# Expert layer in units of 256 rows, with the first layer's weights as the loaded operand

## What is computed

```python
# 1 linear attention with decay, batch 4, heads 8, 768 steps, head size 48
for t in range(S):
    cur = einsum('bhd,bhe->bhde', u*kt, vt)
    y[:, :, t] = einsum('bhd,bhde->bhe', rt, state + cur)
    state = w*state + einsum('bhd,bhe->bhde', kt, vt)
# 2 feed-forward on x [3072, 384]
h = x @ w_in                      # [384, 2048]
x = (h - tanh(h)) @ w_out         # [2048, 384]
# 3 one expert of 8 for each of the 3072 rows, by the largest cosine logit
h = maximum(x[mask] @ w1[e], 0)   # w1 [8, 384, 1024]
out[mask] = gate_w[mask] * (h @ w2[e])   # w2 [8, 1024, 384]
```

## Time and profile before

| | |
|---|---|
| median of three runs | 859.66 us |
| the profiled execution | 856.81 us |
| its span, first to last instruction | 855.0 us |
| granted TensorE clock, mean | 0.993 of 2.4 GHz |
| TensorE busy | 835.6 us (98%) |
| moved by DMA | 179.88 MB |

### The profile page before, as it was taken

One profiled execution on the slowest core, in us unless ns is written; L12 is line 12 of the kernel. 1 busy time (PEld: TensorE's weight loads), 2 busy tenths in 40 slices (PEclk: granted clock), 3 DMA queues, 4 the chain that ended last, 5 costly groups with the idle time before them and its releaser, 6 DMA issues. The chain is left out here.

```text
span 855.0 us, 18997 instructions
## 1 busy us (share of the span) xinstructions
PE 835.6 (98%) x5580; PEld 737.9 (86%) x5581; DVE 557.0 (65%) x886; ACT 481.0 (56%) x1074; POOL 283.3 (33%) x322
## 2 busy tenths in 40 slices
PE   8999989999999999999999999999999999999995
PEld 7777768889998998998998998899988999899984
DVE  8989959999999999999999997411121112111120
ACT  5666777677768777767777765133233323332331
POOL 6244434323443334434433331222222222222211
PEclk9999999999999999999999999899999999999998
DMA  8989943228779768877876986397886386411100
GB/s 245 275 256 298 281 118 95 70 89 281 240 226 298 257 218 272 277 227 257 276 238 224 305 293 226 121 335 281 306 323 249 132 308 217 172 43 46 37 2 1
DMA packets 99386, 179.88 MB, mean 210 GB/s; under 512 B 10267, under 2 KB 25773, under 8 KB 99344
## 3 DMA queue, kind: packets, MB, share of 16 engines
q1 hardware_dynamic: 92016, 163.74, 58.4%
q0 software_dynamic: 3968, 10.82, 3.8%
q10 hardware_dynamic: 3360, 4.79, 1.9%
HBM read 114.83 MB, written 65.86 MB: 211 GB/s over the span
## 5 line engine op out<-in xcount | busy, mean ns | idle before, releaser
L1205 POOL TENSOR_TENSOR ew_l<-ew_raw,ew_h 128x512 fp32r<-128x512 f32 x96 | 126.9, 1329 | 210.0 <-DVE poly L1423 205.7
L1120 PE MATMUL y_ps<-wout_h,g_h 128*128 128x392 f32 x384 | 131.3, 342 | 1.0 <-DVE g_l L1414 0.4
L1121 PE MATMUL y_ps<-wout_l,g_h 128*128 128x392 f32 x384 | 130.4, 340 | 0.0
L1122 PE MATMUL y_ps<-wout_h,g_l 128*128 128x392 f32 x384 | 130.4, 340 | 0.0
L1577 DVE TENSOR_TENSOR ex_hT_l<-e_bank,ex_hT_h 128x512 fp32r<-128x512 f32 x62 | 40.0, 686 | 125.3 <-ACT ex_hT_h L1733 125.3
L1120 PE MATMUL h_ps<-xT_h,win 128*128 (+1 forms) x288 | 113.6, 395 | 1.2 <-DVE diff L1404 0.9
L1304 ACT ACTIVATE g_h<-poly 128x512 fp32r<-128x512 f32 x96 | 61.0, 635 | 94.4 <-DVE poly L1423 93.7
L1122 PE MATMUL h_ps<-xT_h,win 128*128 (+1 forms) x288 | 113.3, 393 | 0.0
L1121 PE MATMUL h_ps<-xT_l,win 128*128 (+1 forms) x288 | 112.8, 392 | 0.0
L1733 ACT ACTIVATE ex_hT_h<-e_bank 128x512 fp32r<-128x512 f32 x62 | 33.8, 597 | 120.2 <-PE e_bank L1647 116.2
L1612 POOL DMA_INDIRECT out_dram<-ex_o_sb,put_i x31 | 31.1, 1002 | 204.1 <-ACT ex_o_sb L1717 204.1
(11 more groups left out here) (188 smaller groups left out, 1826.2 us busy)
## 6 DMA issues: line engine op xcount, KB each, us to landing
ew_raw<-in_w SPq DMA_DIRECT2D x96, 256.0 KB, 3.6
w_h<-ew_h SPq DMA_DIRECT2D x96, 256.0 KB, 3.6
w_l<-ew_l SPq DMA_DIRECT2D x96, 256.0 KB, 2.9
w_ex<-w_h SPq DMA_DIRECT2D x14, 1536.0 KB
w_ex<-w_l SPq DMA_DIRECT2D x14, 1536.0 KB
kv_sb<-in_kv SPq DMA_DIRECT2D x24, 384.0 KB, 5.8
krT_sb<-in_krT SPq DMA_DIRECT2D x44, 192.0 KB, 5.8
x_dram<-xt_sb ACTq DMA_DIRECT2D x48, 96.0 KB, 5.0
```

Source lines behind the costliest of these rows:

```text
L1120: pe.matmul(out, lh, rh, start=start, stop=False)
L1121: pe.matmul(out, lh, rl, start=False, stop=False)
L1122: return pe.matmul(out, ll, rh, start=False, stop=stop)
L1205: pool.tensor_tensor(ew_l[:, slot, :], raw, ew_h[:, slot, :].bitcast(F32), ALU.subtract).then_inc(ew_l_made, 1)
```

## The change

The feed-forward stage no longer splits the experts' first-layer weights. Only the second layer's pieces are split and stored (48 instead of 96: 8 in each middle group, 16 in the last), and `load_first` is gone.

The route builds two kinds of work: 12 **pairs** of 256 rows each and 7 **single tiles** of 128 rows. That needs more small VectorE operations between the count and the tile numbers. `expert_at` is now read by ScalarE inside the route: it loads the raw first-layer weights of pairs 0 and 1 and splits pair 0's, together with GpSimd and VectorE.

In the expert stage TensorE goes through 12 steps, one pair each (`step`). In the first layer of a pair the weights are the loaded operand and the 256 rows stream (L1841 to L1843 of the changed kernel, 72 matmuls of 256 columns). The hidden values come out with rows on columns, so that they need no transposes; ScalarE applies relu and makes the high part in one operation (`hidden_high`), VectorE the low part. The second layer is as before, twice 24 matmuls of 384 columns. Steps 1, 3, 5, 7, 9, 10 and 11 carry a single tile too, which is computed as the tiles before. Each pair's raw first-layer weights (1.5 MB) and each single tile's raw weights of both layers (3 MB) are loaded by DMAs that ScalarE issues, and are split by ScalarE and VectorE in pieces of 128x1024 while TensorE works. SP loads the split second-layer weights of all 8 experts (3 MB each) into two slots, expert 0's from the moment the gates are turned.

```diff
-FETCH = 3
+PAIR = 2 * P
+NPAIR = NT // 2
+NSOLO = E - 1
 SLOTS = 3
+SOLO_SLOT = 2
...
+def load_unit(eng, w_raw, w1, w1_loaded, e, par):
+
+    dst = w_raw[par][:, :]
+    eng.dma_start(dst.rearrange("p (a f) -> p a f", a=NP),
+                  w1[bass.ds(e * NP, NP)].rearrange("a p f -> p a f")).then_inc(w1_loaded[par], 16)
 
 
 def attention(nc, krT, kv, w, u_cols, w_in, w_outT, emb, tau, x_dram, load_group, x_sb, x_stored,
...
-    EXTRA = 4
+    PER = 8
...
             pool.wait_ge(x2_stored, 16 * NT)
             pool.wait_ge(rows_found, 1)
-            pool.indirect_dma_start(rows_sb[:, 0:DM], None, x2_dram,
-                                    bass.IndirectOffsetOnAxis(ap=get_row[:, 0:1], axis=0)).then_inc(gathered[0], 16)
+            for t in range(2):
+                pool.indirect_dma_start(rows_sb[:, t * DM:(t + 1) * DM], None, x2_dram,
+                                        bass.IndirectOffsetOnAxis(ap=get_row[:, t:t + 1],
+                                                                  axis=0)).then_inc(gathered[t], 16)
+            unit_low(pool, 1, w1_first)
...
+            act.wait_ge(h_done, KF * CH)
+            act.wait_ge(units_known, 1)
+            for u in range(2):
+                e = act.value_load(expert_at[0:1, u:u + 1], min_val=0, max_val=E - 1)
+                load_unit(act, w_raw, w1, w1_loaded, e, u)
+            act.wait_ge(w1_loaded[0], 16)
+            for n in range(SPLITS):
+                cols = slice(n * STEP, (n + 1) * STEP)
+                act.activation(unit_h[:, cols], unit_raw[:, cols], ACT.Copy).then_inc(w1_high, 1)
             act.wait_ge(shifted, 1)
             act.activation(ex[:, :, :], below[:, :, :], ACT.Exp).then_inc(ex_made, 1)
...
-            step(dve.scalar_tensor_tensor(out=base[:, :], in0=tend[:, :], scalar=ROUND, in1=ntile[:, 1, :],
-                                          op0=ALU.add, op1=ALU.subtract))
+            later(dve.tensor_scalar(ntile[:, 0, :], count_ps, 1.0 / P, (P - 1) / (2 * P), ALU.mult, ALU.add))
...
+                                    solo_at[:, :].unsqueeze(1).to_broadcast([P, E, E]), ALU.is_ge))
+            later(dve.tensor_reduce(unit_of[:, :], past[0:1, 0:NPAIR, :], AX.X, ALU.add))
+            step(dve.tensor_reduce(skipped[:, :], past_solo[:, :, :], AX.X, ALU.add))
+            dve.tensor_scalar(expert_at[:, 0:NPAIR], unit_of[:, :], float(E - 1), None, ALU.min).then_inc(units_known, 1)
+            later(dve.tensor_tensor(group_at[:, :].rearrange("p (j t) -> p j t", t=2),
+                                    tile_ids[:, :].rearrange("p (j t) -> p j t", t=2), wide(skipped[:, :], 2), ALU.add))
+            step(dve.tensor_tensor(upto[:, :, :], upto[:, :, :],
+                                   pair_rows[:, :].unsqueeze(1).to_broadcast([P, E, E]), ALU.mult))
+            step(dve.tensor_reduce(solo_group[:, :], upto[:, :, :], AX.X, ALU.add))
+            step(dve.tensor_tensor(solo_group[:, :], solo_group[:, :], solo_ids[:, :], ALU.add))
+            step(dve.copy_predicated(group_at[:, ST - E:ST], is_solo, solo_group[:, :]))
...
-            return KF if last else KF + IN_LATE if is_first(g) else KF + EXTRA
+            return KF if last else KF + IN_LATE if is_first(g) else PER
...
-                def load_first(quarter):
-                    sp.wait_ge(h_done, KF * (CH - 1) + FREED * (quarter + 1))
-                    for i in range(MADE):
-                        sp.wait_ge(ew_h_stored[i], 16 * (NP // MADE + 1))
-                        sp.wait_ge(ew_l_stored[i], 16 * (NP // MADE + 1))
-                    part, at = quarter // 2, quarter % 2
-                    for half, src in enumerate((w12_h, w12_l)):
-                        dst = w[:, 0, half, :].bitcast(F32).rearrange("p (s a q f) -> p s a q f", s=2, a=KD, f=PIECE)
-                        pieces_from = src[0:NP].rearrange("(s a q) p f -> s p a q f", s=2, a=KD)
-                        sp.dma_start(dst[:, part, :, at, :], pieces_from[part, :, :, at, :]).then_inc(first_loaded, 16)
 
                 for i in range(MADE):
...
+        def steps(eng, step):
+
+            step(0, 0, 0, None)
+            step(1, 0, 1, 0)
+            with eng.Fori(1, LOOPS) as j:
+                step(2 * j, j, 0, None)
+                step(2 * j + 1, j, 1, j)
+            step(NPAIR - 2, LOOPS, 0, NSOLO - 2)
+            step(NPAIR - 1, LOOPS, 1, NSOLO - 1)
...
+                def load_expert(e):
+
+                    slot = e % 2
+                    if e >= 2:
+                        ends = sp.value_load(ends_at[0:1, e - 2:e - 1], min_val=0, max_val=NPAIR)
+                        sp.wait_ge(tile_done, ends * 2 + 1)
+                    for half, src in enumerate((w2_h, w2_l)):
+                        sp.dma_start(w2_sb[:, slot, half, :].bitcast(F32).rearrange("p (a f) -> p a f", a=NP),
+                                     src[e * NP:(e + 1) * NP].rearrange("a p f -> p a f")).then_inc(w_loaded[slot], 16)
+
+                def pass_expert(e):
...
+                def first(u, par):
+                    high, low = unit_w[par]
+                    if is_first(u):
+                        pe.wait_ge(w1_first, 2)
+                    pe.wait_ge(w1_split, SPLITS * u + 1)
+                    pe.wait_ge(xT_split, 2 * u + 2)
+                    for f in range(KE):
+                        if f % 2 == 0:
+                            wait(pe, hT_split, BLOCKS * u + f // 2 - 1)
+                        ps = h_ps[f // 2 % 2][:, f % 2 * PAIR:(f % 2 + 1) * PAIR]
+                        for a in range(KD):
+                            cols = slice(a * FE + f * P, a * FE + (f + 1) * P)
+                            pe.matmul(ps, high[:, cols], xT_h[:, a, :], start=(a == 0), stop=False)
+                            pe.matmul(ps, high[:, cols], xT_l[:, a, :], start=False, stop=False)
+                            last = pe.matmul(ps, low[:, cols], xT_h[:, a, :], start=False, stop=(a == KD - 1))
+                        if f % 2 == 1:
+                            last.then_inc(hid_done, 1)
...
+                def step(u, j, par, k):
+                    first(u, par)
+                    if k is not None:
+                        transpose_solo(k)
+                    second(u, 0, 0, KE)
+                    if not is_last(u):
+                        transpose_tokens(u + 1, j + par, 1 - par)
+                    if k is None:
+                        second(u, 1, 0, KE)
+                    else:
+                        second(u, 1, 0, KE // 2)
+                        solo_first(k)
+                        transpose_hidden(k, 0)
+                        second(u, 1, KE // 2, KE)
+                        transpose_hidden(k, 1)
+                        solo_second(k)
 
                 pe.sem_inc(tile_done, 1)
...
+                def hidden_high(u):
+                    for i in range(BLOCKS):
+                        act.wait_ge(hid_done, BLOCKS * u + i + 1)
+                        act.wait_ge(tile_done, 2 * u + 1)
+                        act.activation(hT_h[:, 2 * i:2 * i + 2, :].rearrange("p f t -> p (f t)"), h_ps[i % 2][:, :],
+                                       ACT.Relu).then_inc(hT_high, 1)
...
+                def step(u, j, par, k):
+                    hidden_high(u)
+                    load_pair(u + 2, par)
+                    if is_first(u):
+                        load_solo(0)
+                    if k is not None:
+                        solo_x_high(k)
+                        weights_high(k, 0)
+                    finish(u, 0)
+                    if not is_last(u):
+                        for t in range(2):
+                            x_high(u + 1, t)
+                    if k is not None:
+                        weights_high(k, 1)
+                        solo_relu(k, 0)
+                    unit_high(u + 1, j + par, 1 - par, 0)
+                    if k is not None:
+                        solo_relu(k, 1)
+                        solo_hidden_high(k, 0)
+                    unit_high(u + 1, j + par, 1 - par, 1)
+                    if k is not None:
+                        finish(u, 1)
+                        solo_hidden_high(k, 1)
+                    unit_high(u + 1, j + par, 1 - par, 2)
+                    if k is None:
+                        finish(u, 1)
+                    else:
+                        finish_solo(k)
+                        if not (isinstance(k, int) and k == NSOLO - 1):
+                            load_solo(k + 1)
+
+                for t in range(2):
+                    x_high(0, t)
+                steps(act, step)
 
```

625 lines of the change are left out of this document (389 added, 236 removed).

## The result

The changed kernel takes 862.31 us (median of 20 runs, 858.80 to 864.76), the kernel before 855.61 beside it (20 runs). The ratio is 1.0059, with a 95% interval of 1.0038 to 1.0080: slower by some 0.6%, where 853 and the side of "faster" had been forecast. (The ratio is that of the means, 862.32 and 857.29; the kernel before has a tail of runs above 859.) The time lies inside the range of 840 to 870, the direction does not hold.

What follows compares the result with a forecast made beforehand. TensorE was taken to bound both stages. Terms -1 - 18.3 - 2 + 7 + 5.5 + 3.5 = -5.3 us gave 851.5 against the profiled 856.81, moved half way to the median: 853 us, range 840 to 870.

Steps and rivals of the forecast that it cites:

- the side of "faster": Whole kernel: a time below 851.1 us had chance 0.37, within about one per cent 0.45, slower 0.18.
- Steps with a single tile: 0: Expert stage: the single tile's weights are ready with 0.7 and 0.5 to spare; 0 us, ends 0 and +2.5 a step.
- The rival on this side: Single-tile steps: ScalarE becomes the bound, a slip of 2.5 in each of 7 steps, +17.5, time 870; chance 0.17.
- Clock at 1.00 from 560 on: Sign to look for in the changed kernel's profile: TensorE's clock stays full from 560 us on.
- Expert 0's second layer: +3.5: Start of experts: its load, issued once gates are turned, takes 12 us, 8.5 covered; +3.5 us, ends 0 and 6.
- Route: +5.5: Before the experts: more VectorE operations and pair 0's weights delay the first expert matmul; +5.5 us, ends +3 and +9.
- Steps without a single tile: +7: Steps 0, 2, 4, 6, 8: the next first layer waits 1.4 for its split pieces; +7 us, ends 0 and 10.
- First layer of a pair: 0.118: Expert stage: each 256-column matmul takes 0.118 us; with 16 transposes fewer, -1.52 a pair, -18.3 for 12 pairs.
- 0.226: Pairs' first layer, rival: loads do not hide, so 0.226 us a matmul, +93, time 946; chance 0.03.
- Feed-forward: -1: Feed-forward stage: half the splitting goes, at most 2.5 us can come back; -1 us taken.
- 299.4 - 18.3 - 2: Expert stage: 299.4 us before, less 18.3 for the pairs' first layers and 2 for the old stage's two waits.
- The base: Starting time: profiled execution, 2.85 below the median of three runs; 851.5 was moved half way to that median, 853.

Runs made afterwards that it cites:

- Experiment 4: The changed kernel with GpSimd issuing the next single tile's gather ahead of the two scatters, not behind them; 855.5 us, ratio 0.9982 to the kernel before.
- experiments 1 and 6: Each against the changed kernel: 1, VectorE makes two thirds of pair 0's low weights after its gate work, 862.0 us; 6, more `keep_warm` products in the route, 868.75 us.
- experiment 1: The changed kernel with two thirds of pair 0's low weights made by VectorE after its gate work; 862.0 us, ratio 1.0031 to the kernel before.
- experiment 8: The changed kernel with each of GpSimd's 48 low parts of the feed-forward made twice; 903.58 us, ratio 1.0533 to the kernel before.
- Experiment 5: The changed kernel with low parts late, expert 0's second-layer load early, splits early and gather first together; 843.86 us, ratio 0.9835 to the kernel before.

## Why the prediction was wrong

By its own steps:

- **Steps with a single tile: 0.** This is the step that failed. The walk followed ScalarE and the raw weights, found them with 0.5 to 0.7 to spare, and never walked GpSimd's queue: the next single tile's gather stands behind two scatters. In steps 10 and 11, which follow a step with a single tile directly, that is 4.8 us of gaps and 3.1 lost to half clock. Experiment 4 undid the order alone, took 8.2 off these two steps, and got 7.5 back in the sum and 6.8 in the median. Without that error the change would have made no difference that a measurement can tell. The rival on this side had the right steps, but named ScalarE and the raw weights. It came true in step 1 alone: they landed late, and 0.9 us of gaps followed.
- **Clock at 1.00 from 560 on.** Wrong. Three spells of 3.4 us follow three waits, and cost some 1.6 each (two of them are counted above). Step 0 runs its first 72 matmuls at 0.143 a piece and not 0.118, so 1.8 more; the prediction said that this and the wait for the load would not add, and it half holds: experiments 1 and 6, with a faster start, waited longer.
- **Expert 0's second layer: +3.5.** The gap is 4.1, within the ends of 0 and 6, and released by SyncE's queue as foretold; the spell behind it, 1.6, was not counted.
- **Route: +5.5.** Measured 7.8, within 3 to 9. The chain of 23 operations is 3.8 as forecast, and raw weights and table load come in that order. What was missed is GpSimd's low part beside VectorE's operands, 2.7 on one operation, and the half clock behind the barrier; experiment 1 took 2.9 off, 1.4 of it by the clock.
- **Steps without a single tile: +7.** Measured 7.4, at the place and by the releaser that were named.
- **First layer of a pair: 0.118.** Behind step 0 the eleven groups of 72 run at 0.115 to 0.119, 0.117 in the mean: right. A load of 0.19 ahead of each 256-column matmul hides, and no run of this case has anything near 0.226. That speaks against the rule of the Trainium skill's "TensorE: Matmul & The Clock Gate", section "The mechanism", as the prediction put it. The same section also lets a weight load go ahead when it targets the background weight buffer, which the prediction left out and which agrees with these rows.
- **Feed-forward: -1.** Measured -2.1 to -2.3 in the twelve traces with the new feed-forward (all but experiment 8's), near the most that could come back. Where this gain comes from is not shown.
- **What is left.** The items of the expert stage (7.9 and 0.9 in the steps with a single tile, 1.8, 1.6 and 0.6 in step 0, 0.4 in the others) add up to 13.2, 3.9 us more than the 9.3 that it missed by. Experiment 5, whose later steps have no gap, shows where 3.5 of it lie. A step without a single tile takes 17.47 there, one with it 26.97, the last one 26.45: 275.6 for the twelve, where 299.4 - 18.3 - 2 leaves 279.1. A pair saves 1.69 over two tiles of 9.58 and not 1.52. Two errors of opposite sign thus hid a part of each other; that is luck.
- **The base.** The sum says 5.3 less, but 853 is only 2.6 below the 855.61 that 20 runs of the kernel before gave. The prediction went half of the way to the median of three runs, 859.66, which was high. The clock row also has two slices below 9, not one, the second being the last. Neither changes the argument.

The forecast of a small gain thus rested on a right account of TensorE's work, and a walk along too few queues. The gain is there: with the four orders mended the same pair form is 1.65% faster than the kernel before.

## What to carry to other kernels

When a change makes steps shorter or unequal, walk every queue that feeds a step, the scatters and gathers of GpSimd among them, and walk it for two neighbouring steps of the kind that needs most, and for the first such step, not for an average one. Removing one wait among several shows little or nothing until the next is gone as well, so look in the trace where it was given back before giving an edit up: four edits that took 0.6, 2.7, 1.4 and 7.5 us off the sum took 21.0 together. Put the order of gathers and loads by when they are needed, not by the tile that they belong to.
